# A recurrent-attention and routed-MLP kernel: a new order of work inside a chunk, a split first value load, three gather buffers

## The reference, cut to what matters

```python
for t in range(768):                       # attention, per batch and head
    m_new = maximum(f[t] + m, i[t])
    C = exp(f[t] + m - m_new) * C + exp(i[t] - m_new) * outer(v[t], k[t])
    n = exp(f[t] + m - m_new) * n + exp(i[t] - m_new) * k[t]
    y[t] = sigmoid(o[t]) * (C @ q[t]) / maximum(abs(n @ q[t]), 1)
x = y, heads side by side                  # [2, 768, 320]
logits = x @ w_gate;  fresh = argmax(logits[s])
e[s] = fresh if s == 0 or sigmoid(x[s] @ w_local) < 0.5 else e[s - 1]
out[s] = softmax(logits[s])[e] * (relu(x[s] @ w1[e]) @ w2[e])
```

## Time and profile before

| | |
|---|---|
| median of 3 runs | 293.46 us (292.31 to 296.82) |
| profiled execution | 297.23 us, span 295.3 us, mean granted TensorE clock 0.914 |
| TensorE (matmul) busy | 263.5 us, 89% |
| VectorE busy | 176.5 us, 60% |
| ScalarE busy | 123.6 us, 42% |
| GpSimd busy | 64.8 us, 22% |
| DMA | 42.35 MB, 143 GB/s mean |

### The profile page before, as it was taken

One profiled execution on the slowest core, in us unless ns is written; L12 is line 12 of the kernel. 1 busy time (PEld: TensorE's weight loads), 2 busy tenths in 40 slices (PEclk: granted clock), 3 DMA queues, 4 the chain that ended last, 5 costly groups with the idle time before them and its releaser, 6 DMA issues.

```text
span 295.3 us, 5921 instructions
## 1 busy us (share of the span) xinstructions
PE 263.5 (89%) x2097; PEld 197.2 (67%) x2098; DVE 176.5 (60%) x358; ACT 123.6 (42%) x187; POOL 64.8 (22%) x86
## 2 busy tenths in 40 slices
PE   5899699989899899987699599999799999999990
PEld 1577588878788777763236588888676666666560
DVE  6588855397895957977791458888722332233220
ACT  2324634666766847634000346665523222333210
POOL 6073200504104010000021122333223233331111
PEclk9959955999999979996759799999999999999997
DMA  6997562658999881578717148841001010101000
GB/s 149 244 264 280 126 246 71 175 192 255 200 290 288 264 256 30 157 273 267 232 11 269 35 130 266 245 157 51 31 28 35 27 35 13 32 21 45 7 23 19
DMA packets 14305, 42.35 MB, mean 143 GB/s; under 512 B 3795, under 2 KB 5885, under 8 KB 14282
## 3 DMA queue, kind: packets, MB, share of 16 engines
q1 hardware_dynamic: 12314, 37.54, 42.8%
q0 software_dynamic: 1792, 4.34, 4.9%
q10 hardware_dynamic: 176, 0.17, 0.2%
HBM read 38.49 MB, written 4.99 MB: 147 GB/s over the span
## 4 chain that ended last, share of the span: by engine, by line
PE 46%; DVE 6%; DMA 2%; issue 1%; ACT 1%; POOL 0%; POOLq 0%; DVEq 0%
PE psU L927 17%; PE psS L907 9%; PE psO L893 5%; PE psS L893 4%; PE psO L914 2%; PE psS L701 2%; DMA xt<-x_rows,srcid 2%; PE psM L880 2%; DVE W L1220 1%; PE psU L872 1%; PE psM L744 1%; DVE W L1268 1%; PE psS L744 1%; PE psA L854 0%; ACT W L624 0%
## 5 line engine op out<-in xcount | busy, mean ns | idle before, releaser
L927 PE MATMUL psU<-W,hidT 128*128 128x320 f16 (+1 forms) x384 | 54.8, 299 | 0.4 <-DVE hidT L1352 0.4
L927 PEld LDWEIGHTS psU<-W,hidT 128*128 128x128 f16 x384 | 37.5, 98 | 14.7 <-issue 0.9
L788 PEld LDWEIGHTS psO<-W,hidT 128*128 128x128 f32 x192 | 28.1, 210 | 3.0 <-issue 1.1
L907 PE MATMUL psS<-W,xT 128*128 x128 | 28.9, 379 | 0.0
L502 POOL DMA_INDIRECT out<-rows,outid x16 | 16.2, 1010 | 56.7 <-DVE rows L1359 56.7
L766 PE MATMUL psS<-W 104*128 104x256 f32 x96 | 27.9, 428 | 0.0
L1336 DVE TENSOR_TENSOR xT<-psM,xT 128x384 f16<-128x384 f32 x16 | 8.9, 557 | 29.5 <-ACT xT L633 29.5
L633 ACT CAST xT<-psM 128x384 f16<-128x384 f32 x16 | 7.6, 476 | 44.5 <-PE psM L880 44.5
L1094 DVE TENSOR_TENSOR hidT<-psS,hid 128x512 f32<-128x512 f32 x24 | 16.5, 687 | 15.8 <-PE psS L766 15.5
L788 PE MATMUL psO<-W,hidT 128*128 128x41 f32 x192 | 25.9, 287 | 0.0
L468 POOL TENSOR_TENSOR W<-W 128x640 f32<-128x640 f32 x6 | 8.7, 1454 | 75.0 <-PE psU L832 65.0
(11 more groups left out here) (184 smaller groups left out, 480.1 us busy)
## 6 DMA issues: line engine op xcount, KB each, us to landing
W<-in_kvo SPq DMA_DIRECT2D x6, 968.0 KB, 7.2
stage<-in_w SPq DMA_DIRECT2D x9, 640.0 KB, 5.2
stage<-in_w SPq DMA_DIRECT2D x11, 512.0 KB, 4.6
W<-in_w SPq DMA_DIRECT2D x8, 512.0 KB, 5.8
W<-in_w SPq DMA_DIRECT2D x6, 640.0 KB, 5.6
rows<-in_w SPq DMA_DIRECT2D x5, 512.0 KB, 4.5
W<-in_qk SPq DMA_DIRECT2D x6, 416.0 KB
x_rows<-rows SPq DMA_DIRECT2D x12, 192.0 KB, 6.2
```

The costliest lines, as they stand in the source:

```text
L788: last = mm(own[j % 2][:, h], prob[j % 2][:, h], vb[u][:, QUAD * j + h], start=True, stop=True)
L907: last = mm(psS[:, half], x[:, k * P:(k + 1) * P], w, start=(n == 0), stop=(n == len(terms) - 1))
L927: last = mm(psU[:, 0:DM], h[:, k * P:(k + 1) * P], w, start=(k == 0 and n == 0), stop=(k == FC - 1 and n == 2))
```

## The change

- TensorE: `own_part(1)` goes ahead of `scores(2)`, `x_transposes(even)` and `old_part(1)`. In chunk 1 `factors(2, NC)` goes from before `x_transposes` to after `scores(3)`.
- VectorE: `weigh(1)` goes ahead of `make_x`; `make_scale` moves behind `scale_old(1)`; the four `split_low` move to the end: two behind `combine(2)`, two behind the last `keep_logits`. `chunk_decays` is cut in two, `chunk_ends` early, the rest after `weigh(3)`.
- ScalarE: `exponents(1)` and `exponents(2)` each move ahead of a `split_high`; `keep_rows(even)` and `x_evac(odd)` go around the last two `split_high`.
- The values of chunk 0 are loaded ahead of its keys and gates, with a semaphore of their own.
- Static tiles use three gather buffers (`xt` and two parts of `hid`), so gathers 0 to 2 are issued with no wait for a transpose. The late loads from piece 9 on now wait for gather 2.
- 5 late pieces ahead of the tiles, the other 15 over 5 tiles.

```diff
-EARLY_LOWS = 3
-SPREAD_STEPS = 6
+EARLY_LOWS = 5
+SPREAD_STEPS = 5
...
+        xbufs = [xt[:], hid[:, 0:ROW], hid[:, ROW:2 * ROW]]
...
             def load_values(c, u):
+                if c == 0:
+                    sp.dma_start(kvob[u][:, 0:BH * V], kvo[c, :, 0:BH * V]).then_inc(s_v0, 16)
+                    sp.dma_start(kvob[u][:, BH * V:KVO_N], kvo[c, :, BH * V:KVO_N]).then_inc(s_kvo[u], 16)
+                    return
                 sp.dma_start(kvob[u], kvo[c]).then_inc(s_kvo[u], 16)
...
-                    sp.wait_ge(s_xl, 16)
+                    sp.wait_ge(s_xl[2], 16)
...
-            for t in range(3):
+            gather(0)
+            pool.memset(hid[:, 0:2 * ROW], 0.0).then_inc(s_zero, 1)
+            pool.wait_ge(s_zero, 3)
+            for t in range(1, 3):
                 gather(t)
+            for t in range(E - 1):
+                gather(t + 3)
+                write(t)
             n3 = tile_count(pool)
-            with pool.Fori(0, TILES - 3) as t:
+            with pool.Fori(E - 1, TILES - 3) as t:
...
+                exponents(1)
                 if c == 1:
...
                 if c > 0:
                     split_high(A_CHUNK * (c - 1))
-                exponents(1)
+                exponents(2)
                 act.wait_ge(s_kvo[c % 2], 16 * (c // 2 + 1))
                 wait_if(act, s_x, c)
                 nc.scalar.activation(th, ob[c % 2], ACT.Tanh, scale=0.5).then_inc(s_th, 1)
-                if c > 0:
-                    split_high(A_CHUNK * (c - 1) + 1)
-
-                exponents(2)
...
                 else:
                     x_evac(2 * (c - 1))
-                    keep_rows(c - 1, 0)
-                    split_high(A_CHUNK * (c - 1) + 2)
+                    split_high(A_CHUNK * (c - 1) + 1)
                 exponents(3)
                 if c > 0:
+                    split_high(A_CHUNK * (c - 1) + 2)
+                    if c == 1:
+                        act.wait_ge(s_et, 3)
+                    keep_rows(c - 1, 0)
+                    x_evac(2 * (c - 1) + 1)
                     split_high(A_CHUNK * (c - 1) + 3)
-                    x_evac(2 * (c - 1) + 1)
                     keep_rows(c - 1, 1)
                 if c + 1 < NC:
                     stack_queries(c + 1)
...
-                pe.wait_ge(s_kvo[u], 16 * (k + 1))
+                if c == 0:
+                    pe.wait_ge(s_v0, 16)
+                else:
+                    pe.wait_ge(s_kvo[u], 16 * (k + 1))
                 own_part(0)
                 exponents(2)
-                if c == 1:
-                    factors(2, NC)
-                if c > 0:
+                if c == 0:
+                    scores(2)
+                    own_part(1)
+                else:
+                    own_part(1)
+                    scores(2)
                     x_transposes(2 * (c - 1), 0, c - 1)
-                scores(2)
-                if c > 0:
                     old_part(1)
-                own_part(1)
                 exponents(3)
                 if c > 0:
                     logits(2 * (c - 1))
                 scores(3)
...
+                if c == 1:
+                    pe.wait_ge(s_lg, 1)
+                    factors(2, NC)
                 own_part(2)
...
                 weigh(0)
+                weigh(1)
                 make_x(c - 1)
-                split_low(piece)
-                weigh(1)
                 scale_old(0)
                 combine(0)
                 if c == 1:
-                    chunk_decays()
-                make_scale(c - 1)
-                split_low(piece + 1)
+                    chunk_ends()
                 weigh(2)
                 combine(1)
                 scale_old(1)
-                split_low(piece + 2)
+                make_scale(c - 1)
                 keep_logits(2 * (c - 1))
                 weigh(3)
+                if c == 1:
+                    chunk_decays()
                 combine(2)
+                split_low(piece)
...
-                split_low(piece + 3)
+                split_low(piece + 1)
...
                 combine(NQ - 1)
                 keep_logits(2 * (c - 1) + 1)
+                split_low(piece + 2)
+                split_low(piece + 3)
```

More of the change, by code:

```diff
@@ L146, in build @@
         slots = [stage[:, 0], stage[:, 1], over(PIECE)]
-        kb = [v[:, 0:BH * D].rearrange("p (h d) -> p h d", h=BH) for v in kvob]
-        vb = [v[:, BH * D:BH * D + BH * V].rearrange("p (h d) -> p h d", h=BH) for v in kvob]
+        vb = [v[:, 0:BH * V].rearrange("p (h d) -> p h d", h=BH) for v in kvob]
+        kb = [v[:, BH * V:BH * V + BH * D].rearrange("p (h d) -> p h d", h=BH) for v in kvob]
         ob = [v[:, BH * D + BH * V:KVO_N] for v in kvob]
@@ L243, in build @@
         s_pad = sem("split_row_pads_cleared")
+        s_v0 = sem("first_values_loaded")
         s_kvo = [sem(f"values_and_gates_loaded_{u}") for u in range(2)]
@@ L274, in build @@
         s_free, s_fetch = sem("tile_buffer_free"), sem("tile_about_to_be_gathered")
-        s_xl, s_xtr, s_xte = sem("tile_loaded"), sem("tile_transposed"), sem("tile_transposed_kept")
+        s_xl = [sem(f"tile_loaded_{n}") for n in range(3)]
+        s_xtr, s_xte = sem("tile_transposed"), sem("tile_transposed_kept")
         s_meta = sem("tile_meta_kept")
@@ L297, in x_place, with x_buffer, loaded @@
             return psM[:], xT[:]
+        def x_buffer(t):
+            return t % 3 if isinstance(t, int) and t < E else 0
+        def loaded(eng, t):
+            eng.wait_ge(s_xl[x_buffer(t)], 16 * (t // 3 + 1) if isinstance(t, int) and t < E else 16 * (t - E + 4))
         def hidden_of(t):
@@ L482, in gather @@
             def gather(t):
[L484 to L487, removed]
+                if isinstance(t, int) and t <= E + 1:
+                    users = [n for n in range(t) if x_buffer(n) == x_buffer(t)]
+                    wait_if(pool, s_xtr, users[-1] + 1 if users else 0)
+                    wait_if(pool, s_meta, users[-1] + 1 if users else 0)
+                    pool.sem_inc(s_free, 1)
                     rows_of = srcid[:, t:t + 1]
                 else:
+                    pool.wait_ge(s_xtr, t)
+                    pool.wait_ge(s_meta, t)
+                    pool.sem_inc(s_free, 1)
                     pool.tensor_copy(gid[:], srcid[:, bass.ds(t, 1)]).then_inc(s_gid, 1)
-                    pool.wait_ge(s_gid, t - 2)
+                    pool.wait_ge(s_gid, t - E - 1)
                     rows_of = gid[:]
                 pool.sem_inc(s_fetch, 1)
-                pool.indirect_dma_start(xt[:], None, xs[:, :], bass.IndirectOffsetOnAxis(ap=rows_of, axis=0),
-                                        bounds_check=TOK - 1, oob_is_err=False).then_inc(s_xl, 16)
+                pool.indirect_dma_start(xbufs[x_buffer(t)], None, xs[:, :],
+                                        bass.IndirectOffsetOnAxis(ap=rows_of, axis=0),
+                                        bounds_check=TOK - 1, oob_is_err=False).then_inc(s_xl[x_buffer(t)], 16)
             def write(t):
@@ L612, in _ @@
             act.wait_ge(s_lg, NT)
+            act.wait_ge(s_xr, 2 * NT)
             def late_high(n):
@@ L661, in first_step @@
                 if t == E - 1:
+                    act.wait_ge(s_meta, E)
                     relu(E)
@@ L725, in x_transposes @@
                     pe.wait_ge(s_x, x_of + 1)
+                    pe.wait_ge(s_e12, 2)
+                else:
                     pe.wait_ge(s_dec, 1)
@@ L876, in tile_transposes @@
             def tile_transposes(t):
-                pe.wait_ge(s_xl, 16 * (t + 1))
+                loaded(pe, t)
                 wait_if(pe, s_xte, t)
+                x = xbufs[x_buffer(t)]
                 for k in range(KC):
-                    last = nc.tensor.transpose(psM[:, k * P:(k + 1) * P], xt[:, k * P:(k + 1) * P], const("ident"))
+                    last = nc.tensor.transpose(psM[:, k * P:(k + 1) * P], x[:, k * P:(k + 1) * P], const("ident"))
                 last.then_inc(s_xtr, 1)
@@ L1066, in later_gates, with chunk_ends @@
                     assert g[0] == G_A, g[0]
-            def chunk_decays():
+            def chunk_ends():
                 dve.wait_ge(s_e1, 5)
@@ L1075, in chunk_decays @@
                 assert g[0] == G_EG, g[0]
+            def chunk_decays():
                 dve.wait_ge(s_dm, 1)
@@ L1331, in tile_low @@
             def tile_low(t):
-                dve.wait_ge(s_xl, 16 * (t + 1))
-                vv.tensor_copy(ptile[:, bass.ds(t, 1)], xt[:, PCOL:PCOL + 1]).then_inc(s_meta, 1)
+                loaded(dve, t)
+                vv.tensor_copy(ptile[:, bass.ds(t, 1)], xbufs[x_buffer(t)][:, PCOL:PCOL + 1]).then_inc(s_meta, 1)
                 dve.wait_ge(s_xeh, t + 1)
@@ L1416 @@
     ones = np.ones((B, H, S, 1), np.float32)
-    kvo = np.concatenate([by_token(k), by_token(np.concatenate([v, ones], axis=3)), by_token(og)], axis=2)
+    kvo = np.concatenate([by_token(np.concatenate([v, ones], axis=3)), by_token(k), by_token(og)], axis=2)
```

## The result

| | before | after |
|---|---|---|
| median, all executions | 294.69 us (292.31 to 296.82, 4 runs) | 318.31 us (312.32 to 322.78, 4 runs) |
| ratio to before | | 1.065, 95% interval 1.0518 to 1.0783 |
| profiled execution | span 295.3 us, clock 0.914 | span 320.2 us, clock 0.838 |

A later pair of executions gave 316.95 us and a ratio of 1.081 (1.0655 to 1.0967).

What follows compares the result with a forecast made beforehand. Chunks 2, 3 and 5 were taken as TensorE-bound, chunks 0 and 1 as slowed by waits and half clock. Attention +2.0 (-18.4 + 20.4), clock +8.0, tiles -4.4 gave +5.6 us; forecast 300 us, range 288 to 311.

Steps and rivals of the forecast that it cites:

- Chunk 0 and 1: Attention start: the wait for values goes, chunk 0 ends at 22.4 instead of 26.9, chunk 1 at 39.8 instead of 54.8.
- The rival in which this short wait brings the clock down: Chunks 0 and 1: the 0.5 us wait for `weigh(2)` gives back some 8 us; about 308 us, chance 0.10.
- A chunk without stalls: Attention chunks: TensorE's own work is 16.55 us; without stalls x is ready at 111.5 instead of 129.9, -18.4 us.
- The sum: Whole kernel: +2.0 + 8.0 - 4.4 = +5.6 us; 302.8 against the profiled execution, 299.1 against the median, forecast 300.
- The load loop: Chunks 1 to 5: piece p + 3's load waits for a late low; 21.0 us a chunk, stalls 20.4 to 20.8 together.
- The estimate of 3.2 us: Weight loads: a 512 KB piece lands in 3.2 us by the skill's fit, making the stalls about 4 us less.
- The clock: Attention stage: half clock after each of four TensorE gaps of about 4.5 us costs 2.0 a chunk, 8.0 in all.
- The tile stage: Tiles: earlier gather 1, no wait at `first_up(7)`, and a shorter `first_up(1)` sum to -4.4 us, bounds -5.1 and -3.3.
- The hidden load: Attention stage: piece p + 3 has landed when ScalarE wants it, nothing stalls; 270.7 us, chance 0.12.
- The rival of a clock that recovers inside the gap: Attention stage: stalls stay but the half clock costs nothing beyond them; -2.4, about 291 us, chance 0.15.
- The half clock throughout: Attention stage: half clock holds through whole chunks, 8 us a chunk instead of 2, +24; about 320 us, chance 0.08.

Runs made afterwards that it cites:

- four slots: The changed kernel, its order untouched, with a fourth staging slot for weight pieces: 276.64 us, ratio 0.947 to the kernel before.
- the kernel with the filled gap: The changed kernel with 19 filler matmuls ahead of `old_part(0)` in chunks 2 to 5, three slots kept: 292.50 us, ratio 0.9965 to the kernel before.
- the kernel before with late lows: The kernel before with only the first three lows of a chunk moved behind `combine(2)`: 318.88 us.
- the tile part alone: The kernel before with three gather buffers, late loads behind gather 2, five early lows and the rest over five tiles: 292.00 us, ratio 0.987.

## Why the prediction was wrong, by its own steps

**Chunk 0 and 1: right.** Worked out were a wait of 0.5 us for `weigh(2)` and an end of chunk 1 at 39.8; the trace has 0.78 us and 40.0, at the full clock throughout. The rival in which this short wait brings the clock down did not happen: the nine traces with the split load all have the 0.78 us, and in each the clock stays at 1.0 behind it to the end of chunk 0. (The 655 KB behind the values take 2.7 us at 241 GB/s, not 2.5; nothing hangs on it.)

**A chunk without stalls: right.** Worked out 16.55 us; with four slots the pair copies stand 16.5 us apart. Its last x is ready at 113.1, against 111.5 worked out (the terms given, 106.0, 2.9 and 2.4, make 111.3). The sum did not have the wait of 2.17 us for the values of chunk 5: SyncE issues their load only behind that of a piece, which waits for a low that is late now. Issued ahead of it, the values are no longer waited for, but x is ready at 113.1 all the same.

**The load loop: right, and a little too dear.** Worked out 21.0 us a chunk; with the clock held up it is 20.2, 20.2 and 20.5, and 21.0 in the one period at full clock of the changed kernel. The wait of ScalarE and the gap of TensorE (worked out 4.5, measured 4.4 in chunks 2 and 5) are where they were said to be. With the gaps filled the last x is ready at 128.6, 1.3 us earlier than before the change, where the sum had +2.0. One link, the first in chunk 1, from the timelines of VectorE (the low), SyncE (its issue) and the DMA issues (us to landing):

```profile
36.68 1.22 DVE L1245 SCALAR_TENSOR_TENSOR W<-stage,W 128x1024 f16<-128x1024 f32 x1
```

```profile
37.92 0.35 SPq L383 DMA_DIRECT2D stage<-in_w  x1
```

```profile
stage<-in_w SPq DMA_DIRECT2D x1, 640.0 KB, 4.2
```

The low ends at 37.90, the load is issued at 37.92, lands after 4.2, and the high starts at 42.12. The five fourth pieces landed in 3.5, 3.9 and 4.3 us (512 KB) and 4.2 and 4.3 us (640 KB), so the sum did well to go by its rows. The estimate of 3.2 us that it set beside them rests on a fit that the Trainium skill ("DMA: Bandwidth & Descriptors", section Anatomy of one DMA) gives for DMAs issued by GpSimd; these are issued by SyncE.

**The clock: this term failed.** The sum took 2.0 us a chunk, 8.0 in all, "near the shorter stretches", with 8 us a chunk as the far end at a chance of 0.08. Measured against the kernel with the filled gap, chunk by chunk: 28.6 against 20.2, 25.4 against 20.2 and 26.8 against 20.5 are +8.4, +5.2 and +6.3; from the pair copies of chunk 5 to the last x 31.0 against 21.7, +9.3. Sum 29.2 in the traces, 25.8 in the medians, about 20 by the ratios, instead of 8.0. The price for a given length was right: in chunk 3 a stretch of 10.3 us costs 5.2, in chunk 4 13.2 us cost 6.3. The step that was wrong is the choice of length: 2.0 us a chunk stands for a stretch of about 4 us. It was taken near the shorter rows, 3.2 us in the tile stage and 2.7 after two short waits. The row nearest to the case (attention stage, about 3 us idle, 16.5 us at half clock) was left to a rival. In the two traces of the changed kernel the stretches of this stage are 10 to 27 us long, and 40.7 where one ran on into routing. The range did not follow the text either. It says that the end of 8 us a chunk stays for the range, which is +24, but then allows the clock +4 and leaves the rival with +24 out. Why the stretches are this long stays open. Stage and gap alone do not set it: in the kernel before with late lows, gaps of 4.1 to 5.0 us in the same stage were followed by 6.4 to 6.8 us.

With the measured 25.8 in place of 8.0 the sum is +2.0 + 25.8 - 4.4 = +23.4, and 23.6 were measured between the medians. Part of that agreement is luck: the 25.8 comes from the same measurement, and in the traces the loop costs 3.3 us less than the sum had and the clock 29.9 us.

The Trainium skill ("TensorE: Matmul & The Clock Gate", section HAM oscillation) tells of a kernel that waits for a DMA in every tile and starts every tile at the half clock. The first trace of the changed kernel agrees: a half-clock stretch with the wait of each of chunks 2 to 5, and none of them once the gaps were filled. The second agrees in three of the four; in chunk 4, where TensorE did not idle, the clock was back at 102.2 and the period that followed had none. The prediction named this rule as one against the change and then priced it by the mildest rows.

**The tile stage: right.** Worked out -4.4; -4.5 in the traces, and 4.9 with the tile part alone. One part was too careful: the 1.16 us gap ahead of `first_up(1)` brought no half clock back. `first_up(7)` has no wait any more.

**The rivals.** The hidden load did not happen, but four slots make it, and 276.6 is near the 270.7 it was given. The rival of a clock that recovers inside the gap did not happen either; the kernel with the filled gap shows what it would have been worth, 292.5 for 291. The half clock throughout gave 320 (its own +24 makes it 323 to 324) and got 0.08; the measured 318.3 is nearest to this rival. But it was not throughout: of the 25.4 and 26.8 us of chunks 3 and 4, 10.3 and 13.2 ran at half clock.

## What to carry to other kernels

Before moving a cheap instruction to the end of a stage, ask which load waits for its buffer and who wants that load in the same stage: the chain low, issue, landing, high is a loop, and here one more slot removed it with the late order kept. Price a new gap of TensorE by the half-clock stretch that may follow, and let the longest stretch seen in the same stage into the range, not only the short ones; here the half clock cost more than the stall itself, while on the old order about the same gaps brought much shorter stretches. Where the gap cannot be removed, work that computes nothing on TensorE can be worth more than its time.

## What the runs showed of the hardware that was not expected

- A half clock can outlast its cause by far. After 4.4 us idle TensorE was busy for 21.6 of 23.5 us, all at 1.2 GHz. What ends such a stretch in the attention stage after 6.4 us in one kernel, and after 10 or 27 us in two chunks of another, stays open; the runs show only that it varies between kernels and between executions of one program.
- Gaps of 1.90 to 2.37 us four times in a row left the clock at 2.4 GHz in one execution; a gap of 2.37 us in another kernel was followed by 37.5 us at 1.2 GHz, and one of 0.99 us by 10.2 us.
- Removing one short wait early (the values of chunk 0) made the kernel no faster; in the one trace, the slowest of four executions, 27.5 us at half clock followed the next wait, where 16.5 had.
